# A fused attention and two-layer feed-forward kernel: the order of the second products' g_lo parts, and the order of the last tile's Abs and output copies

## The reference

```python
def _moe_ref(x, w_in, w_out):
    h = x @ w_in
    sp = np.where(h > 20.0, h, np.log1p(np.exp(np.minimum(h, 20.0))))
    g = h * np.tanh(sp)
    return (g @ w_out).astype(np.float32)

def _moe2_ref(x, w_in, w_out):       # n_tokens, d_model, d_ff = 3072, 384, 2048
    h = x @ w_in
    g = h * np.cos(h)
    return (g @ w_out).astype(np.float32)
```

## Time and profile before

| | |
|---|---|
| median of 3 runs | 905.66 us (905.63 to 908.57) |
| the profiled execution, its own time | 905.51 us |
| its span, from first to last instruction | 903.8 us |
| mean granted TensorE clock | 0.996 |
| PE busy | 887.9 us (98%) |
| DVE, ACT, POOL busy | 46%, 45%, 40% |

### The profile page before, as it was taken

The page is one execution under the profiler, slowest core; times in us unless marked ns, Lnnn a source line. Parts: engine busy times, 40 slices in busy tenths (PEclk is TensorE's granted clock), DMA queues, the critical chain, the costliest instruction groups (busy, mean ns, idle before and its releaser), DMA issues.

```text
span 903.8 us, 13930 instructions
## 1 busy us (share of the span) xinstructions
PE 887.9 (98%) x5540; PEld 729.4 (81%) x5540; DVE 414.3 (46%) x622; ACT 406.4 (45%) x698; POOL 360.1 (40%) x287
## 2 busy tenths in 40 slices
PE   7899999999999999999999999999999999999997
PEld 6688888888888888888888788888888888888885
DVE  8654322233323222231021666666666575666663
ACT  2443332233223222322354755565655565665654
POOL 7566534344443434343255333333333232323332
PEclk9899999999999999999999999999999999999999
DMA  8554321112111311210032300100200200200000
GB/s 195 162 163 128 92 74 39 39 39 74 39 39 50 94 46 39 74 30 1 36 121 90 100 7 1 70 1 1 70 1 1 71 0 1 71 1 1 35 1 36
DMA packets 17153, 48.13 MB, mean 53 GB/s; under 512 B 2752, under 2 KB 2752, under 8 KB 17088
## 3 DMA queue, kind: packets, MB, share of 16 engines
q1 hardware_dynamic: 17088, 47.23, 18.0%
HBM read 37.79 MB, written 9.44 MB: 52 GB/s over the span
## 4 chain that ended last, share of the span: by engine, by line
PE 53%; issue 29%; POOL 14%; DVE 2%; ACT 1%; DMA 0%; POOLq 0%; ACTq 0%; DVEq 0%
PE bank L378 22%; PE bank L398 22%; POOL g_lo L693 14%; PE bank L315 3%; PE bank L333 2%; PE bank L340 1%; PE bank L345 1%; PE bank L353 1%; PE bank L309 1%; DVE probs L567 0%; DVE suffix L552 0%; POOL shared L706 0%; DMA shared<-aqk_in 0%; DVE growth L559 0%; POOL shared L700 0%
## 5 line engine op out<-in xcount | busy, mean ns | idle before, releaser
L693 POOL TENSOR_TENSOR g_lo<-g,g_hi 128x512 fp32r<-128x512 f32 x192 | 251.9, 1313 | 439.3 <-ACT g_hi L470 439.3
L398 PE MATMUL bank<-g_hi,w_hi 128*128 128x512 f32 x576 | 226.6, 393 | 0.3 <-DVE x_out L606 0.3
L398 PE MATMUL bank<-g_lo,w_hi 128*128 128x512 f32 x576 | 224.5, 390 | 0.7 <-POOL g_lo L693 0.6
L398 PE MATMUL bank<-g_hi,w_lo 128*128 128x512 f32 x576 | 224.3, 389 | 0.0
L470 ACT ACTIVATE g_hi<-g 128x512 fp32r<-128x512 f32 x192 | 120.4, 627 | 110.2 <-PE bank L398 108.5
L378 PE MATMUL bank<-x_hi,w_hi 128*128 128x512 f32 x576 | 165.3, 395 | 0.1
L378 PE MATMUL bank<-x_hi,w_lo 128*128 128x512 f32 x576 | 162.6, 391 | 0.0
L378 PE MATMUL bank<-x_lo,w_hi 128*128 128x512 f32 x576 | 162.4, 390 | 0.0
L398 PEld LDWEIGHTS bank<-g_lo,w_hi 128*128 128x128 f32 x576 | 108.1, 188 | 24.5 <-POOL g_lo L693 1.9
L398 PEld LDWEIGHTS bank<-g_hi,w_hi 128*128 128x128 f32 x576 | 108.1, 188 | 24.5 <-issue 1.1
L378 PEld LDWEIGHTS bank<-x_hi,w_lo 128*128 128x128 f32 x576 | 108.5, 188 | 23.0
(11 more groups left out here) (63 smaller groups left out, 596.4 us busy)
## 6 DMA issues: line engine op xcount, KB each, us to landing
w_raw<-w_in SPq DMA_DIRECT2D x32, 384.0 KB, 3.2
shared<-aqk_in SPq DMA_DIRECT2D x44, 192.0 KB, 3.5
v_sb<-v_in SPq DMA_DIRECT2D x24, 256.0 KB, 4.1
shared<-aqk_in SPq DMA_DIRECT2D x48, 96.8 KB, 3.8
mid<-x_out SPq DMA_DIRECT2D x6, 768.0 KB, 4.9
shared<-mid SPq DMA_DIRECT2D x6, 768.0 KB, 5.5
out<-x_out SPq DMA_DIRECT2D x5, 768.0 KB, 4.0
out<-x_out SPq DMA_DIRECT2D x3, 256.0 KB, 2.4
```

Of the source, the lines that this page charges most:

```text
L398: mm = nc.tensor.matmul(acc[m][:, :], wp[:, f, cols], gp[:, tile % GB, :], start=(f == 0 and n == 0), stop=(f == FT - 1 and n == 2))
L693: nc.gpsimd.tensor_tensor(g_lo[:, tile % GB, :], g[:, tile % GB, :], g_hi[:, tile % GB, :].bitcast(F32), ALU.subtract).then_inc(glo_ready, 1)
```

## The change

Three edits, two of them for the last tiles alone.

1. In `second_product` the nine matmuls of every tile that isn't the first of its block (f > 0, 180 of the 192 tiles) come in another order: first the two g_hi matmuls for m = 0, 1, 2, then the three g_lo matmuls for m = 0, 1, 2. The wait for `glo_ready` now stands in front of the seventh. Tiles with f = 0 keep their order.
2. In ACT's step 192 the Abs of tile 191, cut out of `cosine` into `fold`, goes ahead of `g_part(190)`. In all other steps the order stays.
3. In the last tile each of the three g_lo matmuls increments a new semaphore `last_done`. The copy of accumulator 0 waits for 1, that of accumulator 1 for 2, that of accumulator 2 for 3, in place of all waiting for the end of the tile.

```diff
+                parts = ((w_hi, g_hi), (w_lo, g_hi), (w_hi, g_lo))
+                order = [(m, n) for m in range(KT) for n in range(3)]
+                if f > 0:
+                    order = [(m, n) for m in range(KT) for n in range(2)] + [(m, 2) for m in range(KT)]
+                for i, (m, n) in enumerate(order):
+                    if f == 0 and j > 0 and n == 0:
...
+                    if (m, n) == (0, 2):
+                        pe.wait_ge(glo_ready, tile + 1)
+                    wp, gp = parts[n]
+                    mm = nc.tensor.matmul(acc[m][:, :], wp[:, f, DM + m * P:DM + (m + 1) * P], gp[:, tile % GB, :],
+                                          start=(f == 0 and n == 0), stop=(f == FT - 1 and n == 2))
+                    if tile == 2 * TILES - 1 and n == 2:
+                        mm.then_inc(last_done, 1)
+                    elif i == len(order) - 1:
+                        mm.then_inc(out_done, 1)
...
             def take_acc(j):
-                act.wait_ge(out_done, FT * (j + 1))
+                last = j == 2 * BLOCKS - 1
+                if not last:
+                    act.wait_ge(out_done, FT * (j + 1))
...
                 for m in (0, 2):
+                    if last:
+                        act.wait_ge(last_done, m + 1)
                     nc.scalar.activation(x_out[:, m, :], acc[m][:, :], ACT.Copy).then_inc(acc_act, 1)
...
+                if s == 2 * TILES:
+                    fold(s - 1)
                 if alive(s - 2) and s - 2 >= TILES:
                     g_part(s - 2)
                 if alive(s - 1) and s - 1 >= TILES:
+                    if s < 2 * TILES:
+                        fold(s - 1)
                     cosine(s - 1)
...
             def take_acc(j):
-                dve.wait_ge(out_done, FT * (j + 1))
+                if j == 2 * BLOCKS - 1:
+                    dve.wait_ge(last_done, 2)
+                else:
+                    dve.wait_ge(out_done, FT * (j + 1))
```

More of the change, by code:

```diff
@@ L185, in program @@
         out_done = sem("out_done")
+        last_done = sem("last_done")
         acc_act = sem("acc_act")
@@ L387, in second_product @@
                     pe.wait_ge(sum_ready, 2 * BATCH)
-                for m in range(KT):
-                    if f == 0 and j > 0:
+                parts = ((w_hi, g_hi), (w_lo, g_hi), (w_hi, g_lo))
[4 more added lines that the diff above has]
+                    if f == 0 and j > 0 and n == 0:
                         if m == 1:
@@ L485, in turns, with fold @@
                                      scale=1.0 / TWO_PI).then_inc(u_ready, 1)
-            def cosine(tile):
+            def fold(tile):
                 n = tile - TILES
@@ L491, in cosine @@
                 nc.scalar.activation(here, here, ACT.Abs).then_inc(abs_ready, 1)
+            def cosine(tile):
+                n = tile - TILES
+                here = t[:, tile % 3, :]
                 act.wait_ge(abs_ready, n + 1)
```

## The result

The changed kernel took 905.68 us (median of 14 executions, 903.77 to 907.60), the kernel before on the same chips 907.79 us (14 executions, 905.55 to 909.36): a ratio of 0.9977 with a 95% interval of [0.9967, 0.9987]. So the change gains 0.23%, about 2.1 us by this ratio, where 1.90 us (0.21%) was forecast. But 905.68 lies 0.18 us above the upper end of the range (905.5): not the change, the time it was subtracted from was wrong. Two of the six executions of e5_fill_before, at 974.27 and 1270.70 us with a mean granted clock of 0.867 and 0.655, are left out of all that follows; nothing here shows why they were slow, and no other run had one like them.

The account below looks back on a forecast made before the run. PE, busy 887.9 of 903.8 us, was taken to bound the kernel. 1.44 us from PE's last matmul plus 0.46 us from the copies, 1.90 us off the median of 905.66, gave 903.7 us, range 903.2 to 905.5.

Parts of the forecast that it names:

- The median it started from: Whole kernel before the change: 905.66 us, with undisturbed executions taken to differ by 0.1 to 0.2 us.
- Sum: Whole kernel: 1.44 us from PE plus 0.46 us from the copies, 1.90 us off 905.66, about 903.7 us.
- R3: Rival: a pause between matmuls lowers PE's clock, costing 1.9 us a tile (905.7), or 910.2 and more; chance 0.02.
- The pace in the middle: Steady products before the tail: 0.227 us a matmul, unchanged by the new order; 0 us, at most 2.7 us more.
- R2: Rival: bank changes in the 180 reordered tiles cost 5 ns each, 2.7 us, giving 906.5 us; chance 0.09.
- The three waits for g_lo: Last three second products: PE's weight-load stalls for g_lo go, moving PE's last matmul 1.44 us earlier.
- The close handovers: Last tiles: two operands reach PE with 0.02 to 0.03 us to spare; a miss costs up to 0.11 us.
- The Abs: ACT, tile 191: moved ahead of g_hi of tile 190 at cost 0, it starts Sin and what follows 0.65 us sooner.
- R1: Rival: the Abs doesn't help or close handovers are missed, part of the gain only, 904.2 to 904.8 us; chance 0.12.
- The copies: End of the last tile: copies start as each accumulator completes, moving the stores another 0.46 us earlier.
- R4: Rival: the stores, not PE, are late at the end, so no change is seen, 905.3 to 905.7 us; chance 0.05.
- The new semaphore: Last tile: the semaphore and three increments in place of one cost 0, at most 0.1 us together.

Follow-up runs that it names:

- e5_fill_before: Kernel before, with more throw-away matmuls in four PE pauses of the first 36 us: 903.29 to 905.07 us in the executions kept, ratio to before 0.9958.
- e6: Changed kernel with more throw-away matmuls in four PE pauses of the first 36 us: 901.46 to 903.27 us, ratio to the kernel before 0.9938.
- e11: Changed kernel with 12 in place of 20 throw-away matmuls at the start, lengthening PE's pause before the first scores: 906.91 to 909.25 us in 10 executions.
- e12: Kernel before with six throw-away matmuls in PE's pause at 34 us alone: 903.22 to 907.12 us in 12 executions, ratio to before 0.9977.
- e8: Changed kernel with six throw-away matmuls in PE's pause at 34 us alone: 901.49 to 901.55 us in 4 executions.
- e7: Changed kernel with the second product's three parts outermost, eight bank changes in nine matmuls: second product 2.04 us; tile 189's second product to last store issue 7.51 us.
- e2: Full change without the move of the Abs: 8.04 us from tile 189's second product to the last store's issue (before 9.36, full change 7.51).
- e1: Kernel before with the new matmul order alone: 8.42 us from tile 189's second product to the last store's issue (before 9.36).
- e3: Kernel before with the output copies one by one alone, old matmul order: 8.49 us from tile 189's second product to the last store's issue (before 9.36).
- e4: Kernel before with the move of the Abs alone: 8.84 us from tile 189's second product to the last store's issue (before 9.36).
- e10: Changed kernel with four PE pauses filled by throw-away matmuls and POOL's decay of the state moved behind the weight split: 901.50 to 904.98 us.

## Why the prediction was right or wrong

- **The median it started from: wrong, and this put the time out of the range.** The step that failed is the one in "Sum" that takes 1.90 us off the 905.66 us of three executions, together with the term of the range that says undisturbed executions differ by 0.1 to 0.2 us. Measured over 14 executions, the kernel before has a median of 907.79 and differs by 3.81 us: six lie at 905.55 to 905.74 and eight at 907.69 to 909.36, so 908.57, which the prediction read as a sign that "a median of few runs can lie high", is of the commoner kind. 907.79 - 1.90 = 905.89 would have been 0.21 us from the result. That the three executions missed this was bad luck; that nothing asked why one was 2.9 us off wasn't. The page hinted at it: its row of granted clock has an 8 in the second slice (22.6 to 45.2 us) and 9 everywhere else, and there is the idle time noted before PE's first matmuls (2.02 us at 10.38, 2.03 us at 23.90 and 2.00 us at 36.05). The prediction had the low stretch from 38.62 to 42.60 us in hand, but used it only as the price of a matmul at 0.50 and put no cost or scatter on it. e5, e6, e11 and e12 bear out that the pauses in front of such stretches carry most of the scatter; e8 doesn't fit, and what decides in one execution is open.
- **Its sign for R3 (a 0.5 where the clock was 1.00): it was seen, and means something else.** The profile of after has 0.66 from 10 to 15 and from 25 to 30 us, where before has 1.00. R3 is about a pause that the new order makes, and the first reordered one starts at 53.80 us; from there on the clock is 1.00 in both. e12, on the kernel before, has low stretches at the same two places (0.74 and 0.66) without the change.
- **The size of the gain: right.** 1.90 us forecast; 1.85 in tail length, 1.83 behind tile 0, 1.73 to 1.83 between the lowest times of the pairs (before and after, e5 and e6, e12 and e8), 2.1 by the ratio of 0.9977.
- **The pace in the middle and the 180 reordered tiles at 0: right.** From tile 0's first product to tile 188's second it is 859.79 us before and after; e7 with three more changes of bank a tile adds 0.02 us. R2 and R3 fall. A slip without effect: beside the last three second products there are 177 reordered tiles, not 178.
- **The three waits for g_lo: right, to 0.03 us.** With the frame of before moved by 893.83 - 891.50 = 2.33 us, the forecast has the load for tile 190 at 895.82 (measured 895.82), the first matmul of 191 at 897.99 (898.00) and the last one at 899.83 (899.83, two steps after 899.38). The close handovers held: the one for g_lo of tile 190 was a wait of 0.16 us that moved nothing behind it by more than 0.01 us. The g_hi of tile 191 was in time. The agreement hides one rounding: at the pace of 0.227 us the 26 steps are 5.90 us and not 5.98, so the stalls were 1.54 us before and 0.10 us (6.00 - 5.90) after, where the prediction has 1.46 and 0.02. Both are 0.08 too small, and their difference is 1.44 us either way.
- **The Abs: right.** It found its room (ACT idle for 0.24 us before it, and g_hi of 190 at 895.13, forecast 895.14). R1's price of 0.65 us for its absence was too high; e2 says 0.53. In these rows a weight load begins 0.22 us ahead of its matmul, and a load that waits uses up this lead before it delays anything: in e1 the load is due at 895.65 and begins at 896.27, 0.62 us late, the next matmul is late by 0.62 - 0.22 + 0.11 = 0.51 us (896.61 where 896.10 was due).
- **The copies: 0.46 forecast, 0.38 to 0.41 measured.** ACT's first copy starts at 899.86, 0.09 us behind the end of its matmul (899.38 + 0.39 = 899.77), where 0.04 was taken from before. DVE's starts 0.03 us behind. Why ACT's is later wasn't tried. R4 falls: the stores followed the copies.
- **The new semaphore at 0:** nothing in the rows asks for more; it had no run of its own.

## What to carry to other kernels

Before you subtract a gain from a median, ask how the executions are spread: two clusters 2 us apart, in a program whose granted clock is under 1.00 somewhere, mean that something in it falls one way or the other, and a gain smaller than their distance can only be read inside a trace, from a mark behind the place that scatters to the end. An operand that comes late is best read last by all parts that need it, and a copy that waits for its own part gains most where the parts are complete further apart than the queue behind the copies needs for each. And PE's pauses near the start, while other engines prepare, are worth a try with throw-away matmuls: here six of them in one pause took as much off the kernel before as the whole change (e12, a ratio of 0.9977 for both), and 2.3 us between the lowest times (905.53 and 903.22).

## What the runs showed of the hardware that was not expected

- The same pause doesn't always do the same. Ten profiles have the early pauses unfilled. The first one, ahead of the scores at 10.38 us, was 1.25 to 2.02 us long in five of them (e2, e3, e8, e1, before), and the stretch from 10 to 15 us is at 1.00; it was 2.12 to 4.35 us long in the other five (e12, e4, e7, after, e11), and that stretch is at 0.74 or less. The pause at 22 us was 2.02 or 2.03 us long in all ten: the stretch from 25 to 30 us is at 1.00 in three (before, e1, e8) and at 0.73 or less in seven. The pause at 34 us, 1.96 to 2.01 us long where it wasn't filled (1.37 in e11), was followed by a low clock in all nine such profiles. What decides at 2 us is open.
- The 40 throw-away matmuls at the start took 6.68 us before and 6.14 us after (7.45 in e2), with the same program up to there. They begin slowly and then quicken, at another moment in each execution: from 4.50 to 5.50 us before had 7 of them and after 10, and from 6.50 to 7.50 us both had 11. The view gives a granted clock of 1.00 there all along, so why they begin slowly isn't shown. The length of the pause behind them changes with it (2.02, 2.55 and 1.25 us).
- Three stores of 256 KB issued 0.39 and 0.47 us apart ended 2.9 us after the last issue, issued 0.75 and 0.59 us apart 2.6 us after it (e3).
- One and the same subtraction of 128x768 on DVE took 1.65 us in e6 and 4.69 us in e10, both times beside POOL's work; another of that shape, at 43.55 us in e10 with POOL idle, took 0.95 us. The cause wasn't tried.
